# A fused attention and two-layer expert kernel: packed values of batches 2 to 7 computed on 64-row tiles, with rearranged keys and values, and another beginning of batch 0

## The chip, the cores and the metric

The kernel runs on one core of one Trainium2 chip. The metric is the device time of one execution in microseconds (us), as the median of several executions; lower is better. Everything is float32 in and out; where the kernel needs dense products it splits operands into two fp32r parts (`_hi`, `_lo`) and multiplies in three passes.

## The reference, cut to what matters

```python
def sm_attn(qq, kk, vv):            # softmax(scale * qq kk^T) vv
    s = scale * np.matmul(qq, kk.transpose(0, 1, 3, 2))
    a = np.exp(s - np.max(s, axis=-1, keepdims=True))
    return np.matmul(a / (np.sum(a, axis=-1, keepdims=True) + 1e-09), vv)

p_packed = sm_attn(p, k, v)          # p: 32 packs a head; k, v: 576 keys a head
x = sm_attn(q, p_packed, p_packed)   # 8 batches, 8 heads, 576 tokens, head size 64
x = x / rms(x) * rms_g               # 4608 tokens of 512
x = (silu(x @ w_gate) * (x @ w_val)) @ w_out          # 512 -> 1536 -> 512
out = leaky(x @ w_in, alpha) @ w_out2                 # 512 -> 2048 -> 512
```

The change concerns the second matrix product of `p_packed`: for each of 8 heads, 32 packs by 576 keys times 576 keys by 64.

## The kernel before, in words

Each engine has a hand-written program (`nc.Block`, lines 479 to 1708); they meet through semaphores. The bulk is dense work on TensorE (PE). For each batch `b` there is a tile of the first layer: 24 blocks `i` (12 chunks of hidden units, 2 halves of 288 tokens), each an up part (`up_block`, line 986, three passes at lines 738 to 740) and pieces of the down part. After the eight tiles comes a tile of leftover tokens, then the second layer in a loop of nine tiles.

The attention of batch `c = b + 1` is written between those blocks, at places named in tables (`PE_PLACES`, `DVE_FIRST`, `SECOND`, `LATER` and others, lines 47 to 117). For batch 0 nothing stands beside it: its attention is run off in a straight list of names at the start of each engine's program (PE line 1078, ACT line 1332, DVE line 1677), with `keep_busy` matmuls (line 1071) as many as `FILLERS` (line 122) says before some of the steps. Each of them is one float32 matmul that nothing reads.

The steps of one batch's attention that matter here:

- `scores` (line 755): packs times keys, two halves of 288 keys, with 64 rows and 32 columns of PE each; even and odd heads of a pair lie on partitions 0 to 63 and 64 to 127. Half `h` waits for its keys, `k_in[h]`.
- softmax over keys. For batches 0 and 1 PE turns the weights over (`turn_a`). For batches `c > 1` DVE turns blocks of 32 by 32 (`turn_keys`, line 1414, `a_rows<-a_sb`), and SP moves the result through DRAM (`turn_keys`, line 506): two transfers `a_mid<-a_rows`, one for the even and one for the odd heads, then four `a_keys<-a_mid`, each to 32 partitions, all after both of the first.
- `packed` (line 779) for batches 0 and 1 and `packed_of_keys` (line 800) for the others: 5 chunks of keys, 4 pairs, 2 heads, 40 matmuls with 128 rows, 32 columns and 64 elements moving. Some of the 5 x 128 rows are zeros in `v_sb`. DVE evicts the two results (line 1427), PE turns them over (line 819), ACT evicts that (`pp_t`, line 1161).
- `tokens` (line 830): scores of tokens against the packs (line 837) and products of packs among themselves (line 845). DVE multiplies the latter by a 0/1 mask `own` into the block-diagonal `gram_sb` (`gram`, line 1473). `tokens_ready` (line 821) makes the second half of tokens wait for `gram_set`.
- the softmax over packs on DVE and ACT, `gram` (PE, line 855), `mean`, the norm, and `folded` (line 928), which makes the batch's weights `m_hi`, `m_lo`.

What sets the order around the change: the queues of the engines, each strictly in the order written. On SP, `load_v` (line 495) for batch `c + 1` stands at block 6 of the tile, four transfers for `b > 1`; `turn_keys` stands before the `store_rest` of block 2. On DVE of batch 0 the list runs `turn_s0`, `gram`, `shift0`, `turn_s1`.

A float32 matmul stands as two passes in the trace, so that 40 matmuls are x80 there, and 8 are x16.

Of the kernel before, what the change touches and what calls it, by code (L numbers as in the profile page):

```python
# [13 lines left out]
P = 128  # L14
# [10 lines left out]
KEY_BLOCKS = [(0, 4), (4, 4), (8, 5), (13, 5)]  # L25
assert [at + n for at, n in KEY_BLOCKS] == [at for at, n in KEY_BLOCKS[1:]] + [SEQ // ROWS]
# [95 lines left out]
FILLERS = {"scores0": (5, EARLY_BANK), "turn_a01": (3, EARLY_BANK), "tokens0": (1, EARLY_BANK), "tokens1": (1, EARLY_BANK),  # L122
# [8 lines left out]
def build(nc, q_t, k_t, v_s, p_t, w1_gv, w1_o, w2, rms_g, alpha, out_t):  # L131
# [5 lines left out]
    with ExitStack() as ctx:  # L137
# [29 lines left out]
        q_sb = place("q_sb", [P, PAIRS, SEQ], at=kq_at)  # L167
        v_sb = place("v_sb", [P, CHUNKS, MODEL])
        ae_at = cursor[0]
# [9 lines left out]
        a_keys = place("a_keys", [P, HEADS, CHUNKS, PACK], at=a_t_at)  # L179
# [150 lines left out]
        def pp_ps(c, e):  # L330
            return psum[:, e, 0:HEAD_DIM] if first(c) else psum[:, 3, e * HEAD_DIM:(e + 1) * HEAD_DIM]
# [80 lines left out]
        rows_turned, rows_out, keys_in = sem("rows_turned"), sem("rows_out"), sem("keys_in")  # L412
# [69 lines left out]
        def _(sp):  # L482
# [12 lines left out]
            def load_v(b):  # L495
                if b > 1:
                    for r, (start, n) in enumerate(KEY_BLOCKS):
                        sp.dma_start(v_sb[ROWS * r:ROWS * (r + 1), 0:n, :],
                                     v_s[b][ROWS * start:ROWS * (start + n)].rearrange("(j p) n -> p j n", p=ROWS)).then_inc(v_in, 16)
                    return  # L500
# [5 lines left out]
            def turn_keys(c):  # L506
                for g in range(GROUPS):
                    sp.wait_ge(rows_turned, GROUPS * (c - 2) + g + 1)
                    sp.dma_start(a_mid[g], a_rows[:, g, :]).then_inc(rows_out, 16)
# [117 lines left out]
        def _(pool):  # L627
# [12 lines left out]
            pool.wait_ge(zeroed, PAIRS + 2)  # L640
            nc.gpsimd.memset(v_sb[0:LAST, CHUNKS - 1, :], 0.0).then_inc(consts_set, 1)
# [93 lines left out]
        def _(pe):  # L735
# [64 lines left out]
            def packed_of_keys(c):  # L800

                pe.wait_ge(v_in, 16 * len(KEY_BLOCKS) * c)
                pe.wait_ge(mean_copied, 2 * c)
                pe.wait_ge(m_lo_done, evicted(c))
                pe.wait_ge(keys_in, 16 * len(KEY_BLOCKS) * (c - 1))
# [15 lines left out]
            def tokens_ready(c, h):  # L821
# [312 lines left out]
        def _(act):  # L1134
# [42 lines left out]

            def gram_split(c):
# [44 lines left out]
            def beside(c, name):  # L1223
# [16 lines left out]
                if name == "gram_hi":  # L1240
                    gram_split(c)
# [506 lines left out]
```

## Time and profile before

| what | us |
|---|---|
| median of 3 runs | 1524.96 (1524.94 to 1525.96) |
| profiled execution, its own time | 1525.86 |
| its span, first to last instruction | 1524.0 |
| PE busy | 1513.6 (99%) |
| DVE busy | 726.7 (48%) |
| ACT busy | 444.7 (29%) |
| POOL busy | 193.0 (13%) |
| mean granted clock of PE | 1.000 |

The span and the busy times are of the profiled execution, whose own time is 0.90 above the median of the runs. Busy times of engines overlap; what they leave of the span is idle time, which matters on the engine that sets the end only. In the trace a matmul's end is modelled and its start is recorded.

### The profile page before, as it was taken

How to read it: one execution, taken by the hardware profiler on the slowest of the kernel's cores; microseconds unless marked ns; L12 is line 12 of the kernel's file. 1: busy time of each engine (PE TensorE's matmuls, PEld its weight loads, DVE VectorE, ACT ScalarE, POOL GpSimd, SP SyncE). 2: the span in 40 equal slices, each digit the busy share in tenths (PEclk: the TensorE clock that was granted, in tenths of full speed). 3: DMA queues.
4: the chain of work that ended last, by engine and by line, in shares of the span. 5: the costliest groups of instructions: out<-in, count | busy, mean ns of one | idle time of the engine just before them, and what ended most of it. 6: DMA issues, size and time to landing. Idle time of an engine off the chain costs nothing.

```text
span 1524.0 us, 23354 instructions
## 1 busy us (share of the span) xinstructions
PE 1513.6 (99%) x9430; PEld 1258.5 (83%) x9430; DVE 726.7 (48%) x1234; ACT 444.7 (29%) x789; POOL 193.0 (13%) x197
## 2 busy tenths in 40 slices
PE   8999999999999999999999999999999999999999
PEld 5988888888888888898888888888888888888887
DVE  6674756555564746543443333333333333333333
ACT  4554544534544544422111111111111111111111
POOL 2700000000000000263342020020202001020000
PEclk9999999999999999999999999999999999999999
DMA  9313232130313230242301000010100000010000
GB/s 359 114 42 100 67 99 68 66 101 33 103 36 99 67 98 6 75 136 107 138 1 55 0 28 28 10 47 0 56 0 35 22 28 28 0 55 1 28 0 28
DMA packets 62080, 90.16 MB, mean 59 GB/s; under 512 B 17056, under 2 KB 32416, under 8 KB 61600
## 3 DMA queue, kind: packets, MB, share of 16 engines
q1 hardware_dynamic: 56944, 79.78, 16.5%
q10 hardware_dynamic: 5040, 8.98, 1.5%
q8 instruction: 75, 1.23, 0.3%
q14 instruction: 21, 0.17, 0.0%
HBM read 63.19 MB, written 25.56 MB: 58 GB/s over the span
## 4 chain that ended last, share of the span: by engine, by line
PE 98%; DVE 1%; ACT 0%; DMA 0%; issue 0%; SPq 0%; POOL 0%; POOLq 0%; DVEq 0%
PE psum L738 31%; PE psum L740 30%; PE psum L739 30%; PE psum L934 3%; PE psum L761 1%; PE psum L837 1%; PE psum L810 1%; PE psum L1074 0%; PE psum L866 0%; PE psum L865 0%; PE psum L869 0%; DMA a_keys<-a_mid 0%; PE psum L795 0%; SPq L515 0%; DMA a_mid<-a_rows 0%
## 5 line engine op out<-in xcount | busy, mean ns | idle before, releaser
L1699 DVE TENSOR_TENSOR h_lo<-g,h_hi 128x512 fp32r<-128x512 f32 x144 | 106.5, 739 | 470.2 <-ACT h_hi L1346 470.2
L1346 ACT CAST h_hi<-g 128x512 fp32r<-128x512 f32 x144 | 89.4, 621 | 632.7 <-PE psum L740 599.8
L738 PE MATMUL psum<-an_hi,m_hi 128*128 128x288 f32 x768 | 232.1, 302 | 1.2 <-DVE an_lo L1554 1.2
L740 PE MATMUL psum<-an_lo,m_hi 128*128 128x288 f32 x768 | 225.8, 294 | 0.0
L739 PE MATMUL psum<-an_hi,m_lo 128*128 128x288 f32 x768 | 225.8, 294 | 0.0
L738 PE MATMUL psum<-h_hi,ow_hi 128*128 128x512 f32 (+2 forms) x480 | 182.8, 381 | 0.0
L740 PE MATMUL psum<-h_lo,ow_hi 128*128 128x512 f32 (+2 forms) x480 | 177.7, 370 | 0.0
L739 PE MATMUL psum<-h_hi,ow_lo 128*128 128x512 f32 (+2 forms) x480 | 177.4, 370 | 0.0
L738 PEld LDWEIGHTS psum<-an_hi,m_hi 128*128 128x128 f32 x768 | 144.0, 188 | 24.1 <-issue 14.8
L1655 DVE TENSOR_TENSOR act_sb<-act_sb,psum 128x288 f32<-128x288 f32 x168 | 75.7, 451 | 154.2 <-PE psum L740 136.5
L739 PEld LDWEIGHTS psum<-an_hi,m_lo 128*128 128x128 f32 x768 | 144.3, 188 | 4.2
L740 PEld LDWEIGHTS psum<-an_lo,m_hi 128*128 128x128 f32 x768 | 144.2, 188 | 0.0
L738 PE MATMUL psum<-h_hi,w_hi_front 128*128 128x512 f32 x360 | 140.1, 389 | 0.0
L740 PE MATMUL psum<-h_lo,w_hi_front 128*128 128x512 f32 x360 | 140.1, 389 | 0.0
L740 PE MATMUL psum<-xs,w_hi_front 128*128 128x512 f32 x360 | 140.0, 389 | 0.0
L738 PE MATMUL psum<-xs,w_hi_front 128*128 128x512 f32 x360 | 140.0, 389 | 0.0
L739 PE MATMUL psum<-xs,w_lo_front 128*128 128x512 f32 x360 | 140.0, 389 | 0.0
L739 PE MATMUL psum<-h_hi,w_lo_front 128*128 128x512 f32 x360 | 140.0, 389 | 0.0
L1305 ACT ACTIVATE act_sb<-psum 128x288 f32<-128x288 f32 x168 | 69.0, 411 | 200.7 <-PE psum L740 200.1
L738 PEld LDWEIGHTS psum<-h_hi,ow_hi 128*128 128x128 f32 x480 | 90.2, 188 | 38.2 <-issue 27.3
L1692 DVE TENSOR_SCALAR act_sb<-psum,alpha_sb 128x512 f32<-128x512 f32 x144 | 107.4, 746 | 2.0 <-PE psum L740 2.0
L740 PEld LDWEIGHTS psum<-h_lo,ow_hi 128*128 128x128 f32 x480 | 90.3, 188 | 16.3
(183 smaller groups left out, 2405.6 us busy)
## 6 DMA issues: line engine op xcount, KB each, us to landing
k_sb<-k_t SPq DMA_DIRECT2D x16, 576.0 KB, 5.2
q_sb<-q_t SPq DMA_DIRECT2D x8, 1152.0 KB, 5.5
xs_raw<-y_mid SPq DMA_DIRECT2D x9, 1024.0 KB, 5.2
out_t<-o_sb ACTq DMA_DIRECT2D x34, 256.0 KB, 2.0
gv_sb<-w_gv SPq DMA_DIRECT2D x6, 1024.0 KB, 17.1
w_raw_front<-w SPq DMA_DIRECT2D x10, 512.0 KB, 3.6
v_sb<-v_s SPq DMA_DIRECT2D x12, 320.0 KB, 5.8
a_keys<-a_mid SPq DMA_DIRECT2D x24, 160.0 KB, 3.3
```

The costliest lines, as they stand in the source:

```text
L738: nc.tensor.matmul(dst, w_hi, hi, start=start, stop=False)
L739: nc.tensor.matmul(dst, w_lo, hi, start=False, stop=False)
L740: return nc.tensor.matmul(dst, w_hi, lo, start=False, stop=stop)
L761: mm = nc.tensor.matmul(dst, p_sb[dims, pair, :], k_sb[dims, pair, h * HALF:(h + 1) * HALF], start=True, stop=True)
L810: mm = nc.tensor.matmul(pp_ps(c, e)[PACK * pair:PACK * (pair + 1), :], a_keys[:, e * PAIRS + pair, j, :], v_sb[:, j, head * HEAD_DIM:(head ...
L837: mm = nc.tensor.matmul(s2_ps(e)[PACK * pair:PACK * (pair + 1), :], pp_t[dims, pair, :], q[dims, pair, h * HALF:(h + 1) * HALF], start=Tru ...
L934: mm = nc.tensor.matmul(psum[keys, m_bank(c, j) + e, :].rearrange("p (f n) -> p f n", f=2), pp_tg[dims, pair, :], gv_sb[dims, 2 * j:2 * j ...
L1305: nc.scalar.activation(act_sb[:, s, half * HALF:(half + 1) * HALF], gate_ps, ACT.Silu).then_inc(silu_done, 1)
L1346: nc.scalar.copy(h2_hi[:, f % 2, :], g32[:, f % 2, :]).then_inc(g_hi_done, 1)
L1655: nc.vector.tensor_tensor(dst, dst, val_ps, ALU.mult).then_inc(h32_done, 1)
L1692: nc.vector.tensor_scalar(act2_sb[:, s, :], h, 0.0, alpha_sb[:, f:f + 1], ALU.min, ALU.mult).then_inc(neg_done, 1)
L1699: nc.vector.tensor_tensor(h2_lo[:, s, :], g32[:, s, :], h2_hi[:, s, :].bitcast(F32), ALU.subtract).then_inc(g_lo_done, 1)
```

## The change

1. **Packed values of batches 2 to 7.** The keys of the even heads are laid on partitions 0 to 63 and those of the odd heads on 64 to 127, 9 runs of 64 keys each (`RUNS`, 18 groups of 32 rows in two halves). `packed_of_keys` issues 9 x 4 x 2 = 72 matmuls with 64 rows, 32 columns and 64 elements moving in place of 40 with 128 rows. Their two results go to banks 3 and 2 in place of two ranges of bank 3.
2. **Transfers.** The values of batches 2 to 7 come in a second input array, `v_runs`, in exactly that layout, and `load_v` is one transfer in place of four. The four `a_keys` transfers have pieces of 288 elements in place of 160, and the two for the even heads wait for the first `a_mid` transfer alone (`rows_out` becomes two semaphores).
3. **Beginning of batch 0.** `FILLERS["scores0"]` is 4 in place of 5. `gram` of batch 0 leaves DVE's list: POOL zeroes `gram_sb` at the start, and ACT copies the four diagonal blocks (`first_gram`). The wait for them moves from the second half of `tokens` to the first `folded`.

```diff
-KEY_BLOCKS = [(0, 4), (4, 4), (8, 5), (13, 5)]
+RUNS = SEQ // (2 * ROWS)
+OLD_V = 2
...
-FILLERS = {"scores0": (5, EARLY_BANK), "turn_a01": (3, EARLY_BANK), "tokens0": (1, EARLY_BANK), "tokens1": (1, EARLY_BANK),
+FILLERS = {"scores0": (4, EARLY_BANK), "turn_a01": (3, EARLY_BANK), "tokens0": (1, EARLY_BANK), "tokens1": (1, EARLY_BANK),
...
+        v_rows = place("v_rows", [P, RUNS, PAIRS, HEAD_DIM], at=v_at)
...
-            return psum[:, e, 0:HEAD_DIM] if first(c) else psum[:, 3, e * HEAD_DIM:(e + 1) * HEAD_DIM]
+            if first(c):
+                return psum[:, e, 0:HEAD_DIM]
+            return psum[:, 3, e * HEAD_DIM:(e + 1) * HEAD_DIM] if c == 1 else psum[:, 3 - e, 0:HEAD_DIM]
...
                 if b > 1:
-                    for r, (start, n) in enumerate(KEY_BLOCKS):
-                        sp.dma_start(v_sb[ROWS * r:ROWS * (r + 1), 0:n, :],
-                                     v_s[b][ROWS * start:ROWS * (start + n)].rearrange("(j p) n -> p j n", p=ROWS)).then_inc(v_in, 16)
+                    sp.dma_start(v_rows[:].rearrange("p j q d -> p (j q d)"), v_runs[b - OLD_V]).then_inc(v_in, 16)
...
-                sp.wait_ge(rows_out, 16 * GROUPS * (c - 1))
-                for r, (start, n) in enumerate(KEY_BLOCKS):
-                    dst = a_keys[ROWS * r:ROWS * (r + 1)].rearrange("p h j k -> p h (j k)")
-                    sp.dma_start(dst, a_mid.rearrange("g (q p) n -> p (g q) n", p=ROWS)
-                                 [:, :, ROWS * start:ROWS * (start + CHUNKS)]).then_inc(keys_in, 16)
+                for g in range(GROUPS):
+                    sp.wait_ge(rows_out[g], 16 * (c - 1))
+                    for r in range(2):
+                        at = ROWS * (2 * g + r)
+                        sp.dma_start(a_keys[at:at + ROWS].rearrange("p q j k -> p q (j k)"),
+                                     a_mid[g].rearrange("(q p) n -> p q n", p=ROWS)[:, :, HALF * r:HALF * (r + 1)]).then_inc(keys_in, 16)
...
+            nc.gpsimd.memset(gram_sb[:], 0.0).then_inc(zeroed, 1)
...
-                for e in range(2):
-                    for j in range(CHUNKS):
-                        for pair in range(PAIRS):
-                            head = 2 * pair + e
-                            mm = nc.tensor.matmul(pp_ps(c, e)[PACK * pair:PACK * (pair + 1), :],
-                                                  a_keys[:, e * PAIRS + pair, j, :],
-                                                  v_sb[:, j, head * HEAD_DIM:(head + 1) * HEAD_DIM],
-                                                  start=(j == 0), stop=(j == CHUNKS - 1))
-                    mm.then_inc(pp_mm, 1)
+                for j in range(RUNS):
+                    for pair in range(PAIRS):
+                        for e in range(2):
+                            keys = slice(HEAD_DIM * e, HEAD_DIM * (e + 1))
+                            mm = nc.tensor.matmul(pp_ps(c, e)[PACK * pair:PACK * (pair + 1), :], a_keys[keys, pair, j, :],
+                                                  v_rows[keys, j, pair, :], start=(j == 0), stop=(j == RUNS - 1))
+                mm.then_inc(pp_mm, 2)
...
-                    pe.wait_ge(gram_set, 2 * c + 2)
+                    if not first(c):
+                        pe.wait_ge(gram_set, 2 * c + PAIRS)
...
+                if first(c) and j == 0:
+                    pe.wait_ge(gram_set, PAIRS)
...
+            def first_gram():
+                act.wait_ge(zeroed, PAIRS + 3)
+                act.wait_ge(gram_mm, 1)
+                for pair in range(PAIRS):
+                    rows = slice(PACK * pair, PACK * (pair + 1))
+                    nc.scalar.copy(gram_sb[rows, :, rows], psum[rows, 4:6, 0:PACK]).then_inc(gram_set, 1)
...
-            for name in ("exp0", "exp1", "turn_a1", "packed", "probs0", "fold0",
+            for name in ("exp0", "exp1", "turn_a1", "packed", "gram", "probs0", "fold0",
...
-            for name in ("max0", "max1", "norm0", "turn_a0", "turn_a2", "norm1", "packed", "turn_s0", "gram", "shift0", "turn_s1",
+            for name in ("max0", "max1", "norm0", "turn_a0", "turn_a2", "norm1", "packed", "turn_s0", "shift0", "turn_s1",
```

**DVE, batch 0, from the turning of the first token scores on** (`e_0` is `e2_0`, the scores of tokens, `max` their row maxima). Before:

```order
L1433 STREAM_TRANSPOSE e_0_92<-psum 128x288 [waits s2_mm]
L1433 STREAM_TRANSPOSE e_0_92<-psum 128x288
L1479 TENSOR_TENSOR gram_sb<-psum,own 128x128 [waits gram_mm]
L1479 TENSOR_TENSOR gram_sb<-psum,own 128x128
L1444 TENSOR_REDUCE max_79<-e_0_92 128x18 [waits s2_turned]
L1448 TENSOR_TENSOR e_0_92<-e_0_92,max_79 128x576 [waits max2_done]
```

The same stretch of DVE with the change:

```order
L1448 STREAM_TRANSPOSE e_0_93<-psum 128x288 [waits s2_mm]
L1448 STREAM_TRANSPOSE e_0_93<-psum 128x288
L1459 TENSOR_REDUCE max_80<-e_0_93 128x18 [waits s2_turned]
L1463 TENSOR_TENSOR e_0_93<-e_0_93,max_80 128x576 [waits max2_done]
L1448 STREAM_TRANSPOSE e_0_93<-psum 128x288 [waits s2_mm]
```

Two instructions have left this place. On ACT, in the same stretch of batch 0 with the change:

```order
L1161 COPY a_t<-psum 128x4x128 [waits at_mm]
L1167 COPY pp_t<-psum 128x128 [waits ppt_mm]
L1189 COPY gram_sb<-psum 32x2x32 [waits gram_mm,zeroed]
L1189 COPY gram_sb<-psum 32x2x32 x3
L1178 ACTIVATE e_0_93<-e_0_93 128x576 [waits sub2_done]
```

The four copies at line 1189 are new, between the eviction of `pp_t` and the exponential.

**SP, tile 1, around the transfers of batch 2's keys.** Before:

```order
L531 DMA rest_mid<-act_sb 128x64 [waits h32_done] x2
L509 DMA a_mid<-a_rows 128x576 [waits rows_turned] x2
L515 DMA a_keys<-a_mid 32x8x160 [waits rows_out,y_stored,newton_step]
L515 DMA a_keys<-a_mid 32x8x160 x3
L531 DMA rest_mid<-act_sb 128x64 [waits h32_done] x4
```

With the change:

```order
L512 DMA a_mid<-a_rows 128x576 [waits rows_turned] x2
L519 DMA a_keys<-a_mid 32x4x288 [waits rows_out0,y_stored,newton_step]
L519 DMA a_keys<-a_mid 32x4x288
L519 DMA a_keys<-a_mid 32x4x288 [waits rows_out1]
L519 DMA a_keys<-a_mid 32x4x288
```

The number of transfers is the same; the wait is split in two.

## Rows read from the trace of the kernel before

**Rows 1.** The page: busy time, share of the span and instructions of each engine.
```profile
PE 1513.6 (99%) x9430; PEld 1258.5 (83%) x9430; DVE 726.7 (48%) x1234; ACT 444.7 (29%) x789; POOL 193.0 (13%) x197
```

**Rows 2.** The chain that ended last (start us, us, what), batch 0 and batch 4.
```profile
15.08 0.85 DVE e L1433 x2
...
309.60 3.29 DMA a_keys<-a_mid
```

**Rows 3.** PE's waits, whole span (us, times, longest); its timeline at 28.15.
```profile
PE psum L837 <- DVE gram_sb L1479: 0.8, 1, 0.8
...
28.15 0.40 PE L738 MATMUL psum<-an_hi,m_hi 128*128 128x288 f32 x1 [1.24 <-DVE an_lo L1554]
```

**Rows 4.** Timeline of PE, start of the program; last row from a window at 7.45.
```profile
1.53 4.63 PE L1074 MATMUL psum<-ident,mean_w 128*128 128x256 f32 x10 [1.53 <-POOL ident L631]
6.10 1.78 PE L761 MATMUL psum<-k_sb,p_sb 64*32 64x288 f32 x32
...
7.06 0.82 PE L761 MATMUL psum<-k_sb,p_sb 64*32 64x288 f32 x16
```

**Rows 5.** Instructions on `k_sb` before 12 us, and SP's issues of its two halves.
```profile
L761 PE MATMUL psum<-k_sb,p_sb x32: 403/621/686, 6.1 to 7.5; 64*32 64x288 f32 x32
DMA to landing us min/median/max: 4.2/4.8/5.4
...
0.75 1.02 SPq L489 DMA_DIRECT2D k_sb<-k_t  x2
```

**Rows 6.** Timeline of DVE, ACT and PE, batch 0, around `gram`.
```profile
15.85 0.45 DVE L1479 TENSOR_TENSOR gram_sb<-psum,own 128x128 f32<-128x128 f32 x2
16.22 0.73 DVE L1444 TENSOR_REDUCE max<-e 128x18 f32<-128x576 f32 x1
...
13.86 0.27 ACT L1161 COPY pp_t<-psum 128x128 f32<-128x128 f32 x1 [1.77 <-PE psum L819]
17.78 0.68 ACT L1172 ACTIVATE e<-e 128x576 f32<-128x576 f32 x1 [3.66 <-DVE e L1448]
...
16.45 0.72 PE L837 MATMUL psum<-q_sb,pp_t 64*32 64x288 f32 x16 [0.77 <-DVE gram_sb L1479]
```

**Rows 7.** Timeline of PE around the packed step of batch 3.
```profile
227.16 0.40 PE L740 MATMUL psum<-h_lo,ow_hi 128*128 128x512 f32 x1
227.49 1.32 PE L810 MATMUL psum<-v_sb,a_keys 128*32 128x64 f32 x80
228.74 0.40 PE L738 MATMUL psum<-an_hi,m_hi 128*128 128x288 f32 x1
```

**Rows 8.** The same passes, asked in windows that end at 227.60 and 227.70.
```profile
227.49 0.32 PE L810 MATMUL psum<-v_sb,a_keys 128*32 128x64 f32 x8
227.49 0.43 PE L810 MATMUL psum<-v_sb,a_keys 128*32 128x64 f32 x16
```

**Rows 9.** Passes with 64 rows: windows that end at 233.64, 207.92 and 208.17.
```profile
233.59 0.26 PE L845 MATMUL psum<-pp_t 64*32 64x32 f32 x8
...
207.87 0.45 PE L761 MATMUL psum<-k_sb,p_sb 64*32 64x288 f32 x8
207.87 0.69 PE L761 MATMUL psum<-k_sb,p_sb 64*32 64x288 f32 x16
```

**Rows 10.** Timeline of PE before the packed steps of batches 2 and 4.
```profile
141.80 0.40 PE L740 MATMUL psum<-h_lo,ow_hi 128*128 128x512 f32 x1
142.27 0.26 PE L810 MATMUL psum<-v_sb,a_keys 128*32 128x64 f32 x4
312.36 0.40 PE L740 MATMUL psum<-h_lo,ow_hi 128*128 128x512 f32 x1
313.02 0.27 PE L810 MATMUL psum<-v_sb,a_keys 128*32 128x64 f32 x5 [0.26 <-DMA a_keys<-a_mid]
```

**Rows 11.** SP around batch 4's keys.
```profile
304.76 0.32 SPq L509 DMA_DIRECT2D a_mid<-a_rows  x1
306.91 3.14 SPq L515 DMA_DIRECT2D a_keys<-a_mid  x4
```

More of the change, by code:

```diff
@@ L24 @@
 ROWS = 32
-KEY_BLOCKS = [(0, 4), (4, 4), (8, 5), (13, 5)]
-assert [at + n for at, n in KEY_BLOCKS] == [at for at, n in KEY_BLOCKS[1:]] + [SEQ // ROWS]
+RUNS = SEQ // (2 * ROWS)
+OLD_V = 2
 TOKENS = BATCH * SEQ
@@ L128, with build @@
 SPLIT_AS_USUAL = {0: 1, 1: 2, 2: 3, 3: 4}
-def build(nc, q_t, k_t, v_s, p_t, w1_gv, w1_o, w2, rms_g, alpha, out_t):
+def build(nc, q_t, k_t, v_s, v_runs, p_t, w1_gv, w1_o, w2, rms_g, alpha, out_t):
     y_mid = nc.dram_tensor("y_mid", (P, KC, TOKENS), F32, kind="Internal").ap()
@@ L167, in build @@
         q_sb = place("q_sb", [P, PAIRS, SEQ], at=kq_at)
+        v_at = cursor[0]
         v_sb = place("v_sb", [P, CHUNKS, MODEL])
+        v_rows = place("v_rows", [P, RUNS, PAIRS, HEAD_DIM], at=v_at)
         ae_at = cursor[0]
@@ L178, in build @@
         a_t = place("a_t", [P, CHUNKS, HEADS * PACK])
-        a_keys = place("a_keys", [P, HEADS, CHUNKS, PACK], at=a_t_at)
+        a_keys = place("a_keys", [P, PAIRS, RUNS, PACK], at=a_t_at)
         sq = place("sq", [P, PAIRS, HALF], at=sq_at)
@@ L411, in build @@
         at_act, at_dve = sem("at_act"), sem("at_dve")
-        rows_turned, rows_out, keys_in = sem("rows_turned"), sem("rows_out"), sem("keys_in")
+        rows_turned, keys_in = sem("rows_turned"), sem("keys_in")
+        rows_out = [sem("rows_out0"), sem("rows_out1")]
         pp_copied, ppt_copied, ppg_done = sem("pp_copied"), sem("ppt_copied"), sem("ppg_done")
@@ L508, in turn_keys @@
                     sp.wait_ge(rows_turned, GROUPS * (c - 2) + g + 1)
-                    sp.dma_start(a_mid[g], a_rows[:, g, :]).then_inc(rows_out, 16)
+                    sp.dma_start(a_mid[g], a_rows[:, g, :]).then_inc(rows_out[g], 16)
                 sp.wait_ge(newton_step, 3 * c + 3)
                 sp.wait_ge(y_stored, 32 * (c - 1))
-                sp.wait_ge(rows_out, 16 * GROUPS * (c - 1))
-                for r, (start, n) in enumerate(KEY_BLOCKS):
-                    dst = a_keys[ROWS * r:ROWS * (r + 1)].rearrange("p h j k -> p h (j k)")
-                    sp.dma_start(dst, a_mid.rearrange("g (q p) n -> p (g q) n", p=ROWS)
-                                 [:, :, ROWS * start:ROWS * (start + CHUNKS)]).then_inc(keys_in, 16)
+                for g in range(GROUPS):
[4 more added lines that the diff above has]
+                                     a_mid[g].rearrange("(q p) n -> p q n", p=ROWS)[:, :, HALF * r:HALF * (r + 1)]).then_inc(keys_in, 16)
             def store_y(n):
@@ L800, in packed_of_keys @@
             def packed_of_keys(c):
[L802 removed]
+                pe.wait_ge(v_in, 32 * OLD_V + 16 * (c - 1))
                 pe.wait_ge(mean_copied, 2 * c)
                 pe.wait_ge(m_lo_done, evicted(c))
[L805 to L814 removed]
+                pe.wait_ge(keys_in, 64 * (c - 1))
+                for j in range(RUNS):
[5 more added lines that the diff above has]
+                mm.then_inc(pp_mm, 2)
             def turn_packed(c):
@@ L1176, in a2_split @@
                 nc.scalar.copy(a2_hi[:, h], a2[:, h]).then_inc(a2_hi_done, 1)
+            def first_gram():
[4 more added lines that the diff above has]
+                    nc.scalar.copy(gram_sb[rows, :, rows], psum[rows, 4:6, 0:PACK]).then_inc(gram_set, 1)
             def gram_split(c):
-                act.wait_ge(gram_set, 2 * c + 2)
+                act.wait_ge(gram_set, 2 * c + PAIRS)
                 nc.scalar.copy(flat(gram_hi[:]), flat(gram_sb[:])).then_inc(gram_hi_done, 1)
@@ L1239, in beside @@
                     a2_split(c, int(name[-1]))
+                if name == "gram":
+                    first_gram()
                 if name == "gram_hi":
@@ L1725 @@
         "k_t": heads_t(k),
-        "v_s": v.transpose(0, 2, 1, 3).reshape(BATCH, SEQ, MODEL),
+        "v_s": v[0:OLD_V].transpose(0, 2, 1, 3).reshape(OLD_V, SEQ, MODEL),
+        "v_runs": v[OLD_V:].reshape(BATCH - OLD_V, PAIRS, 2, 2, RUNS, ROWS, HEAD_DIM).transpose(0, 2, 3, 5, 4, 1, 6).reshape(
+            BATCH - OLD_V, P, RUNS * PAIRS * HEAD_DIM),
         "p_t": p.reshape(BATCH, PAIRS, 2, PACK, HEAD_DIM).transpose(0, 2, 4, 1, 3).reshape(
```

## The prediction

> **What bounds the kernel now.** I read the page first: PE is busy 99% of the span and nothing else reaches half [rows 1]. So time can only come from PE's own work, from the about 10 us in which PE is idle, or from what delays PE's dense stream as a whole. The chain of waits says the same: it is PE's dense stream from 28.15 to the end, and before that the attention of batch 0, which stands beside nothing, so that a microsecond there is a microsecond of the kernel. In that beginning the chain runs over DVE [rows 2]; PE waits once for `gram_sb` and last for `an_lo` [rows 3]. I then read the timeline of PE at each place that the change touches: the start [rows 4, 5], `gram` of batch 0 [rows 6], the packed steps [rows 7 to 10], and SP's transfers of keys [rows 11]. Everything edited lies either in the first 17 us or in six packed steps of 1.25 us. Against 1525 us this is little, and the question is the sign and the tenths.
>
> The sum is made against the profiled execution (1525.86) and its differences carried over to the median of the runs (1524.96). About 0.2%, 3.05 us, is what a measurement of this kernel can tell from no change.
>
> **One filler less before the first scores.** Ten passes of fillers run from 1.53 on and end at 6.16; the first scores start at 6.10 [rows 4]. One filler is two passes, 4.63 x 2 / 10 = 0.93 with the ends counted, about 0.85 by pace, so the first half could start at about 5.24. Its keys allow that: the first transfer of `k_sb` is issued at 0.75 and takes 4.2 to land, 4.95 [rows 5]. The second half is what counts, since the maxima need both. It started at 7.06 [rows 4], behind the first half, which took 0.96. Its keys are issued at about 1.3 and take 5.4: they land at about 6.7 [rows 5]. So the first half is over at about 6.2, PE idles some 0.6 us, and the second half starts at about 6.8: 0.26 gained, not 0.85. The transfer is what is late next. Less of it remains at the end: the passes of the scores took up to 686 ns at first and 403 at last [rows 5], that is, PE came to its full pace during the second half. If that comes at the same moment as before, an earlier half does more of its work at the slow pace. Bounds 0 and 0.26; I take **0.13**, their middle.
>
> **`gram` of batch 0 off DVE.** The two masked products occupy DVE from 15.85 to 16.22 [rows 6], on the chain between the turning of the scores and their maxima: 0.37 leaves. The second half of the token scores was held for them until 16.45 [rows 6]; now it waits for the first turnings alone, 15.93 by 15.08 + 0.85 [rows 2], and starts at about 16.05. DVE wants it only after the maxima (0.73 [rows 6]) and a subtraction of that size, at about 17.3, and it takes 0.72 [rows 6], so it stays hidden. ACT takes the four copies after the products of packs, which PE starts before DVE turns the scores at 15.08 [rows 2], and next has the exponential at 17.78, before which it idled 3.66 us [rows 6]. The nearest row for a small copy from PSUM is the 0.27 of `pp_t` [rows 6]; four are at most 1.1, so `gram_sb` is there at about 16.2, while the first fold that now waits for it can't start before the token scores end at 16.6. If a copy took twice as long, the fold would slip by 0.6, and it has slack. POOL's added memset lies among the memsets of the start, ahead of everything that needs the keys at 4.95. Gain **0.37**, bounds 0.2 and 0.4.
>
> **The packed step.** Before, 80 passes: by two windows, 8 more passes start in 0.43 - 0.32 = 0.11 [rows 8], four each 56 ns, as there are four column tiles. 20 rounds are 1.12; from the first pass to the next dense matmul it is 228.74 - 227.49 = 1.25 [rows 7], so 0.13 is the way in and out. After, 144 passes over eight tiles of 64 x 32. That eight of these run side by side is seen: the scores' passes come eight at a time, and the next eight add 0.69 - 0.45 = 0.24 [rows 9] for 288 elements, which is 53 ns for 64. That eight can be started that fast is seen too: eight passes of the products of packs start within a window of 0.055 [rows 9]. So 18 rounds of 56 ns, 1.01, plus 0.13, plus 0.03 for four more starts in the first round: 1.17. Gain 0.08 a batch, six batches: **0.50**. Bounds: no more than 2 rounds, 0.11 x 6 = 0.67. On the other side stands the pace of a pass so far, 1.10 / 80 = 13.8 ns, at which 64 more passes cost 0.88 a batch, 5.3 in all. I take the first, because the rows of the same tile shape say so; what they don't show is such a pace kept up over 72 matmuls, only over 8 to 16. This is the largest unknown.
>
> The Trainium skill speaks against the change here: "TensorE: Matmul & The Clock Gate", section "Wait — 56ns, not 53.3ns?", says that the start of one matmul never follows another by less than about 25 ns, however small. By it, 64 added passes would cost 1.6 us a batch, an estimate of 9.6 us in all. The trace does not agree: passes start 13.8 ns apart over a whole packed step and about 7 apart within a round.
>
> **The keys' transfers.** In batches 3 and 5 to 7 the step follows its predecessor without a stall: 227.49 - 227.16 = 0.33 [rows 7]. In batches 2 and 4 the same distance is 0.47 and 0.66 [rows 10]: 0.14 and 0.33 of waiting for `a_keys`, **0.47** in all. In batch 4 the second `a_mid` transfer is issued at 304.76, the four key transfers from 306.91 on take SP 3.14 [rows 11], and the last lands at 309.60 + 3.29 = 312.89 [rows 2]. With the change the first two can go some 0.8 earlier, before the second `a_mid` lands, and only two stand behind it; pieces are 1152 bytes in place of 640, half as many. That is at least 0.8 earlier where 0.33 is wanted. Bounds 0 and 0.47. `load_v` as one transfer frees SP of three issues a batch, in another part of the tile and well ahead of its use, which hides it; nothing.
>
> **Sum.** 0.13 + 0.37 + 0.50 + 0.47 = 1.47, so 1524.4 for an execution like the profiled one and **1523.5** for the median. What follows the beginning keeps its distance: the transfers of weights for the first layer were not what PE waited for, and I take it that 0.5 earlier they still are not; if one were, it would take back part of the 0.50 of the beginning.
>
> **Rivals.**
>
> *The 64-row passes don't keep the pace* (slower). PE's feed or the weight loads, twice as many for the same work, hold a long run at the old 13.8 ns a pass, as would also happen if the two row halves took turns. For it: no row shows 72 small matmuls on end, and four tiles were never asked for more than four passes in 56 ns. Against it: [rows 9]. The step becomes 1.25 + 0.88 = 2.13, 0.96 over the forecast, six times 5.8: 1529.3. It decides the sign from 12.2 ns a pass on: 1528.0 is 4.5 over the forecast, 0.75 a step, so a step of 1.92. Chance 0.07.
>
> *Every start costs a floor* (slower, and the rule above as a rival). As a mechanism of this step it would be that a start can't follow the one before it by less than some fixed time; [rows 8, 9] show 56 ns for four starts and less than 0.055 for eight, so the floor is no more than 7 ns and 144 passes need 1.0 at it, which is the forecast. By the skill's 25 ns the time would be 1523.5 + 0.5 + 9.6 = 1533.6. Chance 0.01.
>
> *A pace in between*, 8 to 9 ns: a step of 1.3 to 1.45 in place of 1.25, so that the packed part loses 0.3 to 1.2 where it should gain 0.50. 1524.3 to 1525.2. Chance 0.15.
>
> *The beginning doesn't gain.* PE has a hole of 0.6 us before the second half of scores and comes to its full pace later. The first half of scores took 0.96 at the slow pace, twice the 0.48 of the later pace; one or two more pieces of such size at half pace cost 0.5 to 1.0 and turn the 0.50 into a loss of up to 0.5: 1524.0 to 1524.5. Chance 0.15.
>
> *More than 3 us gained* would need a wait to go that no row shows. Chance 0.02.
>
> **How the numbers follow.** The forecast has 0.60; the middle rivals have 0.15 each. Of all cases only the first two rivals (0.07 + 0.01) leave the 3.05 us on the slow side: faster 0.02, within 0.2% 0.60 + 0.15 + 0.15 = 0.90, slower 0.08. The range: all gains at their upper bounds are 0.26 + 0.40 + 0.67 + 0.47 = 1.80, 1523.2, less 0.6 since the runs shown lie up to 1.0 apart: 1522.6. Upwards the two middle rivals together give 1525.4 to 1525.7; 1525.8.
>
> **What would show it.** The packed step of 144 passes lasting 1.17 from its first pass to the next dense matmul, eight passes each 56 ns; the distance before it 0.33 in all six batches; `a_keys` landing a microsecond or more earlier relative to it; the second scores starting at 6.8 behind a DMA wait; the maxima 0.4 closer behind the turned scores; the first dense matmul at about 27.65 in place of 28.15. A packed step over 1.25 breaks the largest term; a first dense matmul no earlier than before breaks the beginning.

## The result, and the profile after

| | before | changed |
|---|---|---|
| median of 20 runs each, us | 1525.32 (1524.70 to 1525.96) | 1527.72 (1527.34 to 1529.48) |
| profiled execution, its span | 1525.86, 1524.0 | 1527.63, 1525.8 |
| a second profiled execution (e10, e13) | 1525.73, 1523.8 | 1528.31, 1526.5 |

The ratio is 1.0018, its 95% interval 1.0011 to 1.0024: the changed kernel is slower, by the medians 2.4 us. The prediction said 1523.5, at most 1525.8.

The page of the changed kernel, busy time of PE, and the queues that carry the engines' programs:

```profile
PE 1515.2 (99%) x9812; PEld 1259.2 (83%) x9812; DVE 722.9 (47%) x1232; ACT 445.6 (29%) x793; POOL 192.8 (13%) x198
...
q8 instruction: 78, 1.28, 0.4%
q14 instruction: 22, 0.18, 0.0%
```

PE has 382 more passes than [rows 1] (384 were added, and the filler's two are gone) and is busy 1.6 longer. Before, q8 had moved 75 pieces.

Timeline of PE, changed kernel, around the packed steps of batches 3 and 5 (start us, us, what):

```profile
226.69 0.40 PE L745 MATMUL psum<-h_lo,ow_hi 128*128 128x512 f32 x1
227.02 1.91 PE L815 MATMUL psum<-v_rows,a_keys 64*32 64x64 f32 x144
228.85 0.40 PE L743 MATMUL psum<-an_hi,m_hi 128*128 128x288 f32 x1
...
398.06 0.40 PE L745 MATMUL psum<-h_lo,ow_hi 128*128 128x512 f32 x1
398.38 1.66 PE L815 MATMUL psum<-v_rows,a_keys 64*32 64x64 f32 x144
399.97 0.40 PE L743 MATMUL psum<-an_hi,m_hi 128*128 128x288 f32 x1
```

In batch 5 the step takes 399.97 - 398.38 = 1.59 where it took 1.25 [rows 7]. So it is in batches 4 to 7; in batch 3 it takes 1.84, in batch 2 1.78. Before, all six took 1.254 (start of the first pass to the next dense matmul, from the trace). The distance in front of it is 0.33 in all six: the waiting of [rows 10] is gone. The last keys land 1.2 to 2.1 before PE reaches the step, by the trace; in the kernel before it was from 0.9 before to 0.2 too late.

The beginning, PE, then DVE and ACT around `gram`, then the first dense matmul:

```profile
1.53 3.78 PE L1080 MATMUL psum<-ident,mean_w 128*128 128x256 f32 x8 [1.53 <-POOL ident L635]
5.24 1.21 PE L766 MATMUL psum<-k_sb,p_sb 64*32 64x288 f32 x16
6.75 0.76 PE L766 MATMUL psum<-k_sb,p_sb 64*32 64x288 f32 x16 [0.29 <-DMA k_sb<-k_t]
...
14.69 0.85 DVE L1448 STREAM_TRANSPOSE e<-psum 128x288 f32<-128x288 f32 x2 [1.64 <-PE psum L841]
14.91 0.89 ACT L1189 COPY gram_sb<-psum 32x64 f32<-32x64 f32 x4 [1.18 <-PE psum L849]
15.57 0.75 DVE L1459 TENSOR_REDUCE max<-e 128x18 f32<-128x576 f32 x1
...
17.39 1.09 PE L940 MATMUL psum<-gv_sb,pp_tg 64*32 64x512 f32 x16 [1.08 <-DMA gv_sb<-w_gv]
...
27.51 0.40 PE L743 MATMUL psum<-an_hi,m_hi 128*128 128x288 f32 x1 [1.24 <-DVE an_lo L1569]
```

The second scores start at 6.75 behind the keys' transfer, as forecast (6.8). DVE's turning starts 0.39 earlier than in [rows 2], and the maxima 0.65 earlier than in [rows 6]; the first dense matmul comes at 27.51, 0.64 earlier than in [rows 3]. ACT has the four copies done at 15.80. So the beginning gained, the stalls went, and still 2.4 us were lost: in the six packed steps, and, as it turned out, at the very end.

### The profile page after: what moved, and what is told of

The parts are those of the page before. It is cut to its first block, busy times and chain, and to the rows that moved or that the text cites. A ratio compares the mean times of both kernels' runs of the same rounds, so it can differ in the third digit from the quotient of the medians.

```text
span 1525.8 us, 24103 instructions
## 1 busy us (share of the span) xinstructions
PE 1515.2 (99%) x9812; PEld 1259.2 (83%) x9812; DVE 722.9 (47%) x1232; ACT 445.6 (29%) x793; POOL 192.8 (13%) x198
## 4 chain that ended last, share of the span: by engine, by line
PE 98%; DVE 1%; DMA 0%; ACT 0%; issue 0%; SPq 0%; DVEq 0%
PE psum L743 31%; PE psum L745 30%; PE psum L744 30%; PE psum L940 3%; PE psum L815 1%; PE psum L841 1%; PE psum L766 1%; DMA k_sb<-k_t 0%; PE psum L870 0%; PE psum L873 0%; PE psum L869 0%; PE psum L800 0%; PE psum L780 0%; PE psum L904 0%; PE psum L905 0%; ACT a_sb L1152 0%
```

## The experiments: which part costs

Two theories after the result. *Supply*: PE's program can't be handed on as fast as eight tiles can work, so 72 small matmuls wait for their instructions. *Tiles*: the row halves take turns, or the eight tiles have a slower pace of their own. First, each part of the change alone.

**e1**: the kernel before with the new beginning only (4 fillers, `gram` on ACT). **e2**: the changed kernel with the beginning of before.

> The kernel before with only the changed beginning of batch 0 (four fillers, the diagonal blocks of batch 0 copied by ACT). Theory A, the traces add up: the first dense matmul 0.64 us earlier, the packed steps as before (1.25 us each, stalls before batches 2 and 4), so 0.6 us faster, 1524.7. Rival B, the part of the slowdown that the profile of the change does not show (about 1 us of its 2.4) comes from the new beginning in unprofiled executions: then no gain or up to 1 us slower.

> The changed kernel with the old beginning (five fillers, DVE makes the diagonal blocks). Theory A: the six packed steps with their waits cost 1.9 us over before, so about 1527.3 to 1528.4 (0.64 over the changed kernel). Rival B: at or below the changed kernel's 1527.7, since the beginning was what cost.

e1 took 1526.20, ratio 1.0003 (0.9994 to 1.0012); e2 1528.56, 1.0020 (1.0011 to 1.0029). Only e2 is clear of noise: that loss is in the packed part. For the new beginning alone no gain is seen, and its interval allows one of 0.9 as well as a loss of 1.8. PE's last matmul starts 0.11 earlier than before, though e1 waited 0.49 for the keys of batch 4, but behind that matmul the kernel went on for 4.30 us instead of 3.68. I come back to that end.

**e3** halves the elements that move, **e4** puts each of the 72 matmuls on all 128 rows, so that there are no row halves. Both leave out half of each head's 64 values, and e4 also mixes the two heads of a pair.

```diff
# e3, in packed_of_keys of the changed kernel (e4: [:, pair, j, :] and [:, j, pair, 0:32])
-mm = nc.tensor.matmul(pp_ps(c, e)[...], a_keys[keys, pair, j, :], v_rows[keys, j, pair, :], ...)
+mm = nc.tensor.matmul(pp_ps(c, e)[..., 0:32], a_keys[keys, pair, j, :], v_rows[keys, j, pair, 0:32], ...)
```

> The changed kernel, but each packed matmul of batches 2 to 7 moves 32 of its 64 elements, so half of the packed values of these batches is not computed. Feed theory (PE gets matmuls no faster than about one in 17 to 20 ns after the first 16): first to last pass stays 1.44 us, since the number of matmuls is the same. Tile theory (each tile is busy 56 ns a pass, something in it slows eight tiles): it falls to about 0.95 us or less. Rival: row halves read or write in each other's way, then also shorter, about 0.8 to 1.1.

> The changed kernel, but each of the 72 packed matmuls takes all 128 rows and moves 32 elements, so the packed values of batches 2 to 7 are sums over both heads' keys and half of them is missing. No row halves remain. Feed theory: 1.44 us again from first to last pass, as 72 matmuls are issued. Row-half theory: the slow stretch goes and the step is at the pace of four tiles, 36 rounds of 27 to 30 ns, 0.97 to 1.1 us.

Their steps in batch 5, then how many passes of e3 have started by 398.35 and by 398.85:

```profile
397.82 1.42 PE L815 MATMUL psum<-v_rows,a_keys 64*32 64x32 f32 x144
399.17 0.40 PE L743 MATMUL psum<-an_hi,m_hi 128*128 128x288 f32 x1
...
397.82 0.72 PE L815 MATMUL psum<-v_rows,a_keys 64*32 64x32 f32 x61
397.82 1.22 PE L815 MATMUL psum<-v_rows,a_keys 64*32 64x32 f32 x121
```

```profile
398.97 1.61 PE L814 MATMUL psum<-v_rows,a_keys 128*32 128x32 f32 x144
400.51 0.40 PE L743 MATMUL psum<-an_hi,m_hi 128*128 128x288 f32 x1
```

With half the elements moving the step is still 1.35, and without row halves 1.54. From first to last pass they take 1.23 and 1.42, by the trace. *Supply* had said 1.44 for both, *tiles* at most 1.1: e4 is near the first, e3 lies between. But in e3 60 passes start in 0.50: 8.3 ns apart, 16.7 for a float32 matmul, although half as many elements move. In e4 passes 40 to 64 start in 0.20, the same 8.3. It isn't the row halves. The times, 1527.11 (1.0012, 1.0003 to 1.0022) and 1527.80 (1.0015, 1.0006 to 1.0025), fit the steps.

**e5** cuts the 72 matmuls into 40 and 32, with six dense matmuls between them.

```diff
-    "PE": {(0, "between", 7): ["packed"], (0, "after", 8): ["turn_packed"],
+    "PE": {(0, "after", 7): ["packed_a"], (0, "between", 7): ["packed"], (0, "after", 8): ["turn_packed"],
```

> The changed kernel with its packed step cut in two: runs 0 to 4 (40 matmuls, 80 passes) in front of the six down matmuls of block 7, runs 5 to 8 (32 matmuls, 64 passes) behind them. Theory of the supply (the first 16 small matmuls stand ready and run eight passes in 56 ns, the rest arrive one in about 19.5 ns): each piece gets its own 16 ready ones, so from first to last pass 0.22 + 24 x 0.0195 = 0.69 and 0.22 + 16 x 0.0195 = 0.53, together 1.22 against 1.444 in one piece; with the way out and in paid twice the kernel takes about the same time as the changed one, 1527.7. Rival (row halves or tiles slow each other from the beginning, 20 ns a matmul throughout): 0.80 and 0.64, together 1.44, and the kernel takes 0.26 x 6 = 1.6 more, 1529.3.

It took 1530.15 (1.0032, 1.0020 to 1.0044), and the pieces 0.82 and 0.64: the numbers of the rival, not mine. Yet the starts inside them rule the rival out as well, since they are those of the uncut step. From the trace, when every eighth pass starts (ns, batch 5 of the changed kernel; first piece of e5 at 398.21; e7, below):

```
pass          0    8   16   24   32   40   48   56   64   72
changed       0   80  135  191  266  414  480  547  625  725
e5, piece 1   0   80  136  192  267  415  481  548  625  726
e7            0   40   72  100  228  295  361  428  495
```

The first eight passes take 80 ns, as the first rounds did before; from then on eight go in 56 ns, the pace that was forecast, up to about pass 32. Then comes a hole, and then 67 ns for eight (8.3 ns a pass), with a further hole of some 30 ns now and then.

The hole is in the weight loads too. Of the loads of this step, those that have started by 398.65, 0.27 behind the first:

```profile
398.38 0.30 PEld L815 LDWEIGHTS psum<-v_rows,a_keys 64*32 64x32 f32 x33 [0.36 <-issue]
```

By 398.60 there were as many. So loads and passes are missing together. Nor are the loads themselves what takes 8.3 ns: the first 33 start 6.6 ns apart inside a round, and those of e7 (below) 3.3 ns apart, which rules out a pace set by the loads. For e5 I had counted the saving of the ready passes in a new piece but not the hole behind them, which comes again in each. With the way in and out paid twice, e5 is slower still.

**e7** asks in what the supply is counted. Each matmul takes only the upper 16 bits of both operands, so one load and one pass in place of two and two.

```diff
# in the matmul of packed_of_keys, cut to its two operands
-... a_keys[keys, pair, j, :], v_rows[keys, j, pair, :] ...
+... a_keys[keys, pair, j, :].bitcast(mybir.dt.bfloat16)[:, 1::2], v_rows[keys, j, pair, :].bitcast(mybir.dt.bfloat16)[:, 1::2] ...
```

> The changed kernel, where each of the 72 matmuls takes only the upper 16 bits of its keys' weights and values (as bfloat16), so that it is one load and one pass instead of two of each. The lower half of both operands is left out. Measured so far: in the steps of 144 passes the starts go eight in 56 ns up to pass 32, pause 0.15, and then go eight in 67 ns (16.7 ns a float32 matmul), whether 64 or 32 elements move and with 64 or 128 rows. If the supply is counted in instructions (a load and a pass each, four a float32 matmul), the 72 passes take from first to last about 0.5 to 0.65. If it is counted in matmuls, 16.7 ns each, they take about 1.2 as with half the elements moving. Last matmul of the kernel: by the first 6 x 0.85 = 5 earlier than with the change, by the second 6 x 0.25 = 1.5 earlier.

Its step in batch 5, with the passes started by 395.40, 395.57 and 395.70:

```profile
395.21 0.75 PE L815 MATMUL psum<-v_rows,a_keys 64*32 64x64 bf16 x72
395.89 0.40 PE L743 MATMUL psum<-an_hi,m_hi 128*128 128x288 f32 x1
...
395.21 0.32 PE L815 MATMUL psum<-v_rows,a_keys 64*32 64x64 bf16 x32
395.21 0.55 PE L815 MATMUL psum<-v_rows,a_keys 64*32 64x64 bf16 x48
395.21 0.68 PE L815 MATMUL psum<-v_rows,a_keys 64*32 64x64 bf16 x64
```

The same 72 matmuls take 0.68 instead of 1.59. Sixteen passes start in 0.13 again, 8.3 ns each, and each is now a whole matmul. The hole again follows 32 passes, now 32 matmuls. So the supply is counted in instructions, a load and a pass each, and neither in matmuls nor in elements: about 32 pairs stand ready in front of the array, the next comes 0.23 (e7) to 0.30 (e4) behind the first pass, and after it a pair comes every 8.3 ns. What in PE makes it 8.3 isn't shown. The Trainium skill, "Advanced Engine Details and Errata", section "Engine Queue Depths", gives TensorE's queue a depth of 64, "complicated with tiling"; 32 loads and 32 passes are 64, so the trace agrees. One run took 1521.96.

## The experiments: batches 2 and 3, the stalls, and the end

**e10** and **e13** are the two kernels once more, for a second profiled execution of each.

> The kernel before, unchanged, for a second profiled execution. The stalls in front of the packed steps of batches 2 and 4 were 0.14 and 0.33 in the first, and 0 to 0.49 in kernels that don't touch them; the first dense matmul was at 28.15, and at 27.81 in a kernel whose beginning is the same. If these are chance of an execution, this one differs from the first by tenths of a microsecond in both, the packed steps are 1.254 and the tail is 3.73 again. If they belong to the program, all figures repeat.

> The changed kernel, unchanged, for a second profiled execution. Besides 1.444 from first to last pass in every batch it lost 0.19 behind pass 143 in batch 2 and 0.25 behind pass 130 in batch 3. If PE stands there at the end of a 16 KB piece of its program whose successor hasn't landed, the same two passes show a gap again, of another size, and it ends 2.2 to 2.6 after the start of the last transfer on the queue of instructions; the tail is 4.3 and the 8 KB transfer lies 2.3 behind the last matmul again. If they are chance of an execution, the gaps are gone or lie elsewhere. The first dense matmul may differ by tenths, as it did between two executions of the kernel before (28.15 and 28.27).

The kernel before, at its first dense matmul and in front of batch 2's packed step:

```profile
28.27 0.40 PE L738 MATMUL psum<-an_hi,m_hi 128*128 128x288 f32 x1 [1.23 <-DVE an_lo L1554]
...
141.85 0.40 PE L740 MATMUL psum<-h_lo,ow_hi 128*128 128x512 f32 x1
142.52 1.32 PE L810 MATMUL psum<-v_sb,a_keys 128*32 128x64 f32 x80 [0.27 <-DMA a_keys<-a_mid]
```

The stall is 0.67 - 0.33 = 0.34 in batch 2 and none in batch 4, where it had been 0.14 and 0.33 [rows 10]. Stalls for keys belong to the kernel, their places and sizes to one execution; in e1b, which touches no transfer of keys, there was none. With the transfers of the change there is none in any of seven executions (the changed kernel twice, e2, e3, e4, e5, e7).

The changed kernel again, batch 3:

```profile
227.10 1.50 PE L815 MATMUL psum<-v_rows,a_keys 64*32 64x64 f32 x131
228.77 0.34 PE L815 MATMUL psum<-v_rows,a_keys 64*32 64x64 f32 x13 [0.17 <-issue]
229.03 0.40 PE L743 MATMUL psum<-an_hi,m_hi 128*128 128x288 f32 x1
```

The gap lies behind pass 130 (counted from 0) as in the first execution, 0.39 where it was 0.29, and in batch 2 the last pass is again followed by 0.33 instead of 0.15. e3 and e4 have their gaps behind the same two passes (0.49 and 0.40; 0.27 and 0.69). e2, whose program has one filler more in front and so two passes more, has its large one behind pass 128 (0.64). So it is a place in PE's program. q8 moves that program in pieces of 16 KB, 75 before and 78 now: three pieces of 16 KB are 49,152 bytes, and the change adds 6 x 32 matmuls of four instructions, 768, which makes about 64 bytes each and 256 to a piece. The trace bears this out: PE's loads, passes and semaphore instructions from the gap of batch 2 to the gap of batch 3 number 1537 in both executions and 1536 in e2, and six pieces are 1536. In these five executions (the changed kernel twice, e2, e3, e4) a piece starts on q8 0.3 to 0.9 before the step of batch 3, and the gap ends 2.2 to 2.6 behind that start. A packed step of 72 matmuls is 288 instructions, more than a piece holds. By that count the ends of two pieces fall into the step in batches 2 and 3, less than 1.5 us apart, and of one in batches 4 to 7, where no such gap is. e5 has small gaps at the same places of batches 2 and 3 and one of 0.12 in its batch 4, again about 6 x 256 instructions on, where its cut step begins just behind the end of a piece. So where PE runs through a whole piece before the next one is in, it stands. That last link is inferred from these times and counts; no run changed the pieces. The Trainium skill, "Advanced Engine Details and Errata", section "ISA Cache", has lines of 16 KB for 256 instructions; the size of the pieces and the count agree.

**e1a** and **e1b** are the two halves of the new beginning alone.

> The kernel before with four fillers instead of five, and nothing else of the change. The new beginning as a whole (e1) moved the first dense matmul from 28.15 to 27.92 and not the time. If one filler less is a real gain, the maxima of the scores come about 0.3 to 0.4 earlier, the first dense matmul comes at about 27.8 and the time is 0.3 below the kernel before (1525.0). If a cold or late start gives it back (rival), the first dense matmul is at 28.0 to 28.3 and the time is not below 1525.3. The tail behind the last matmul is 3.7 if it does not hang on the beginning, 4.3 if this part of the beginning is what lengthened it.

> The kernel before with gram of batch 0 copied by ACT instead of masked by DVE, and nothing else of the change. If the path runs over DVE as forecast, the first dense matmul comes 0.2 to 0.4 earlier (27.75 to 27.95) and the time is 0.2 to 0.4 below the kernel before. If the wait of the first fold for weights from memory takes its place, the first dense matmul stays at 28.1. The tail behind the last matmul is 3.7 if it does not hang on the beginning, 4.3 if this part is what lengthened it.

Neither moves the time beyond noise, and 0.3 couldn't be seen in it: 1525.45 and 1525.52, both 1.0001 (0.9992 to 1.0010). The first dense matmul came at 27.82 and 27.52, but it lay at 27.81 in e6 too, whose beginning is the old one, and at 27.92 in e1. One execution differs from another by as much as these edits should give. Taken over all 17 profiled executions the two parts come apart. From DVE's turning to the first dense matmul it is 13.07 (13.06 to 13.08) in the nine with `gram` on DVE and 12.83 (12.82 to 12.84) in the eight with it on ACT. The turning itself starts at 14.91 in the mean of the nine with five fillers (14.57 to 15.21) and at 14.73 with four (14.49 to 15.08). So `gram` gives 0.24 and the filler about 0.17, less than its spread. Another thing that doesn't vary is the end. The last matmul of the kernel, by the timeline of PE, before:

```profile
1520.27 0.39 PE L740 MATMUL psum<-h_lo,w_hi_back 128*128 128x512 f32 x1
```

and in e1b:

```profile
1519.09 0.39 PE L741 MATMUL psum<-h_lo,w_hi_back 128*128 128x512 f32 x1
```

With spans of 1524.0 and 1523.4 the end behind it is 3.7 against 4.3. Eight profiled executions have 3.7 (before twice, e1a, e2, e6, e8, e11, e12), all without the copies on ACT; the eight with them (the changed kernel twice, e1, e1b, e3, e4, e5, e7) have 4.3.

**e9** tests whether that is the length of ACT's program: the kernel before with four copies more on ACT, which nothing reads.

```diff
+                    for pair in range(PAIRS):
+                        nc.scalar.copy(spare[:, pair, :], ident[:, 0:PACK])
```

> The kernel before with four copies of 32 columns more on ACT, which nothing reads, where the changed kernel has its four copies of gram. In all kernels with gram on ACT the last output lands 0.6 later after the last matmul (tail 4.3), and an 8 KB transfer on the queue of instructions lies at 2.3 after the last matmul, among the last output's packets; in all others it lies at 4.7 and the tail is 3.7. If the length of ACT's program decides where that transfer falls, this kernel has it at 2.3 and a tail of 4.3. If it is DVE's or POOL's program, it stays at 4.7 and 3.7.

Its last matmul, and the DMA queues from 1522.0 to 1524.3:

```profile
1520.00 0.39 PE L740 MATMUL psum<-h_lo,w_hi_back 128*128 128x512 f32 x1
```

```profile
q1 hardware_dynamic: 144, 0.26, 29.8%
q10 hardware_dynamic: 28, 0.02, 3.3%
q14 instruction: 1, 0.01, 0.8%
```

The span is 1524.3, so the end is 4.3, and the piece of program on q14 lies among the last output's packets, 2.3 behind the last matmul; in the kernel before it comes 4.6 behind it, when all is over. The output's last packets end 3.36 behind the last matmul, where it was 2.87. So 0.6 of the loss comes from four small instructions on ACT at the beginning, 1500 us away. That they do it by shifting where a piece of a program ends fits the times, but is inferred. The delay by this one packet is larger than the packet (0.31), and why isn't shown.

## The experiments: the search for a version that beats both

**e6**: the kernel before, keys in eight transfers of four heads, the first four behind the first `a_mid`.

> The kernel before, its packed step of 40 matmuls with 128 rows unchanged, with the keys sent in eight transfers of four heads each instead of four of eight heads, the first four behind the first a_mid transfer alone. It is the candidate that should beat both kernels: it takes the one part of the change that helped and leaves the 72 matmuls out. Theory: the packed step stays 1.254 in all six batches, the distance before it is 0.327 in all six, the last matmul comes 0.47 earlier than in the kernel before, time 1524.9. Rival: eight issues hold SP as long as before or longer, so that the last keys land no earlier and the stalls of 0.14 and 0.33 stay: time 1525.3.

It took 1525.39, 1.0001 (0.9992 to 1.0010). Batch 2 had no stall, batch 4 still 0.14, where SP's eight issues took 4.82. Half a microsecond at most is in it, and this can't be told from nothing.

**e8** puts only the last 64 keys on half-height tiles, so that no row holds a zero and there are still 40 matmuls; **e12** runs those first.

```diff
# cut to the line that picks the rows
+                            keys = slice(0, P) if j < CHUNKS - 1 else slice(HEAD_DIM * e, HEAD_DIM * (e + 1))
```

> A candidate that should beat both kernels. Keys again on all 128 rows in four chunks (32 matmuls), and only the last 64 keys of each head on 64 rows, even heads on partitions 0 to 63, odd heads on 64 to 127 (8 matmuls side by side): 40 matmuls in place of 72, and 80 passes in 18 rounds of 56 ns, since no row holds a zero. Values come in one transfer in that layout, keys in eight transfers; the beginning is that of the kernel before. Theory (the step is bounded by the array as long as a matmul has more than 16.7 ns, 28 here): first to last pass 1.105 - 0.11 = 1.0, to the next dense matmul 1.14, all six; distance before the step 0.327; the tail 3.7. Gain 0.11 x 6 = 0.67 and up to 0.47 of stalls: 1524.2 to 1524.8 against 1525.3. Rival: the change from full-height to half-height tiles drains the array, each of the two turns costs some 0.06 and takes the round back: 1.25, 1524.9 to 1525.4.

> As the kernel with keys on all 128 rows in four chunks and the last 64 keys of each head on 64 rows (e8), with the eight half-height matmuls first instead of last. There the turn from full height to half height took 225 ns for eight passes instead of 112, and the step 1.303 instead of 1.254. If only that turn costs, since a tile of half height waits for the array to drain, the turn now lies behind the dense matmul, where the array drains anyway, and the step is 1.15 to 1.20: below both kernels. If every change of height costs, also from half to full, it is 1.30 again.

```profile
397.53 1.37 PE L813 MATMUL psum<-v_sb,a_keys 128*32 128x64 f32 x80
398.83 0.40 PE L740 MATMUL psum<-an_hi,m_hi 128*128 128x288 f32 x1
```

```profile
397.97 1.37 PE L813 MATMUL psum<-v_sb,a_keys 64*32 64x64 f32 x80
399.27 0.40 PE L740 MATMUL psum<-an_hi,m_hi 128*128 128x288 f32 x1
```

Both steps are 1.30, so the rival of e8 held, with a higher price than its 0.06 a turn, and e12's theory fell. By the starts of rounds (passes side by side) in the trace, the turn from full to half height costs 0.11, 170 ns to the next round instead of 56; the turn back costs 0.14, 192 ns instead of 56. The round behind a turn then takes 80 ns instead of 56, some 0.02 more. The times are 1525.90 (1.0004, 0.9995 to 1.0013) and, in one run, 1526.20. The Trainium skill, "TensorEngine Tiling (Array Packing)", section "Key Properties", says that a change of tiling mode drains the array; the trace agrees, with these 0.11 and 0.14.

**e11** is e7's edit in the step of before.

> The kernel before, its packed step of 40 matmuls on 128 rows, where each matmul takes only the upper 16 bits of its keys' weights and values (as bfloat16): one load and one pass, 40 of each. The lower half of both operands is left out. With one pass each, 72 matmuls took 0.553 from first to last pass and 0.682 to the next dense matmul, bound by the supply of instructions behind pass 32. If that supply is the limit, 40 passes are nearly all standing ready: 32 of them run at the array's pace (four in 28 ns, 0.22) and eight follow at 8.3 ns behind a pause, 0.35 to 0.40 from first to last, about 0.5 to the next dense matmul. That is 0.75 a batch less than the kernel before and 0.2 less than 72 matmuls: 1520.8 for the kernel. Rival: a floor per step of some 0.13 a round of four, as in the first eight passes, gives 0.6 and more.

```profile
396.02 0.50 PE L810 MATMUL psum<-v_sb,a_keys 128*32 128x64 bf16 x40
396.45 0.40 PE L738 MATMUL psum<-an_hi,m_hi 128*128 128x288 f32 x1
```

The step is 0.43, 0.25 shorter than with 72 matmuls, and has no hole, where one had been expected: passes start about 7.8 ns apart on average, so that the one behind the first 32 isn't due before 0.25, and in e7 it had come at 0.23. The time is 1521.48, ratio 0.9970 (0.9959 to 0.9982), 4.4 below the kernel before on that chip, although three of its steps waited 0.97 in all for keys. Only this version and e7 (one run, 1521.96) are clearly below both kernels, and both give up precision: this product is made from 16-bit halves. In full float32 nothing tried here is clearly faster than the kernel before. A version of e11 whose keys land earlier, as they do with the change, would have these 0.97 to gain at most; it wasn't run.

## Why the prediction was wrong, point by point

**Packed step: the term that failed**, forecast as a gain of 0.50, measured as a loss of 0.34 x 6 = 2.0 and another 0.4 to 0.5 in the gaps of batches 2 and 3. The failed sentence is that 144 passes take 18 rounds of 56 ns, because [rows 9] show such a pace over 8 to 16 passes. They do, and it is kept for about 32 passes; behind them it is 67 ns for eight, with holes. [rows 9] showed the array working on what stood ready, and I took it for what PE can be fed. A step of 80 passes at 13.8 ns never asked for more than the supply has. My first rival named the feed but priced it with 13.8 ns, which was the array's pace on four tiles, so that it gave 2.13 for the step; measured is 1.59. The rival in between stopped at 9 ns and 1.45; the pace was 1.444 / 144 = 10.0.

**The 25 ns between starts** that the Trainium skill gives ("TensorE: Matmul & The Clock Gate", section "Wait — 56ns, not 53.3ns?") don't hold here, as the prediction said: passes start about 4 ns apart over e7's first 24 and 8.3 apart when supplied. But the direction of that rule was right: with 32 elements moving instead of 64 (e3), a pass behind the first 32 still costs 8.3 ns.

**Stalls**: forecast 0.47. They are gone in both executions of the changed kernel, by the mechanism that was forecast: the keys land 1.2 to 2.1 ahead. In the kernel before they were 0.48 and 0.34 in its two profiled executions, so the forecast size rests on one execution and was right for it.

**Filler**: forecast 0.13; the turning came 0.39 earlier, most of it the chance of one execution, since over all executions it is about 0.17. **`gram`**: forecast 0.37; from the turning to the maxima it is 0.88 where it was 1.14 [rows 2, 6], 0.26, and 0.24 of it are left at the first dense matmul, within its bounds. So the beginning is worth about 0.4 where 0.50 was forecast; that the first dense matmul came at 27.51 and 27.52 against 28.15 and 28.27, 0.7 in the mean, is in part luck. What I took for certain and was not is that this reaches the end: with the copies on ACT the end grew by 0.6, which no term had.

**Sum** with the mean of two executions each: 2.0 + 0.5 (gaps) + 0.6 (end) - 0.4 (stalls) - 0.7 (beginning) = 2.0. The profiled executions differ by 2.2 in the mean, the medians by 2.4. Some 0.4 of e13 arose behind its last packed step, most of it spread evenly over the second layer (400 passes take 90.72 there instead of 90.67), and is not traced to anything.

**The chances**: 0.90 lay on a change within 0.2%, and 2.4 us is within it. That part held because everything edited is small beside 1525 us; it says nothing for the mechanism, whose sign was wrong.

## What to carry to other kernels

Splitting a small product over more tiles multiplies instructions, and the supply has its own pace, which a short burst in a trace doesn't show. Before doing it, count loads and passes: here, beyond the first 32 passes, no step of 72 or 144 passes had them closer than 8.3 ns apart, so 64 more passes cost more than fewer rounds could save. Half a microsecond in 1525 also hangs, as far as these runs show, on where pieces of the programs end, so an edit at the beginning has to be judged at the last output and not at the first dense matmul, and one trace of each kernel isn't enough to see such a size.

## What the runs showed of the hardware that was not expected

- Float32 matmuls of 2 passes are supplied one in 16.7 ns, one-pass matmuls one in 8.3 ns (e3, e4, e7), after about 32 load-and-pass pairs that stand ready (0.27 with 64 float32 elements moving). The hole behind them is 0.09 to 0.1 in the changed kernel and e7, and comes once in each piece of e5. The smaller holes of some 30 ns stay open; the changed kernel, e4 and e5 have them, e3 and e7 don't.
- A change from 128-row to 64-row tiles inside a step costs 0.11, the change back 0.14 (e8, e12).
- PE stood 0.1 to 0.7 longer than usual at two fixed places of its program, 6 x 256 instructions apart, in line with pieces of 16 KB that can be used 2.2 to 2.6 after their transfer starts.
- Four small instructions more on ACT at 15 us lengthened the end by 0.6 (e9, and all kernels with `gram` on ACT).
